# Bucketed attention, a routed expert layer and a dense layer: the third tile pair of each attention group split over two groups

## The chip, the cores and the metric

One core of a Trainium2 chip runs the whole program in one launch. The metric is the device time of that launch in microseconds (us). The kernel before took 792.55 us in the median of three runs (791.42 to 792.79).

## The reference

Three layers follow each other.

```python
# attention: 2 x 8 heads, 768 tokens, 64 wide
q_bucket = sum(((q @ proj) > 0) * 2**arange(6))      # the same for k
scores = where(q_bucket == k_bucket, q @ k.T / 8, -1e9)
attn = exp(scores - max(scores)); attn /= sum(attn) + 1e-9
x = attn @ v                                          # 1536 tokens x 512
# expert layer: 8 experts, the best one of each token, 512 -> 1024 -> 512
# dense layer: 512 -> 2048, ELU, -> 512
```

The change touches the attention alone.

## The kernel before

The work is written out by hand for each engine, with semaphores between the engines. `GROUPS` = 54 groups `n` are run; `g = n // 3` is the head that is being prepared and `part = n % 3` the third of it. Below, "head group g" means the three parts of one g. In its three parts TensorE prepares head g, takes the scores of head g-1 and applies the weights of an older head to v. The steady head groups are g = 2 to 15; g = 16 and the two parts that follow (n = 51, 52) only finish what is under way, and the document calls them the drain.

A head has six query tiles of 128 rows, numbered through all heads as `m`. In part p of head group g the tiles `m_s` and `m_s + 1` get their scores, with `m_s = 2 * (n - 3)`, and the tiles `m_e = m_s - 2` and `m_e + 1` have their exponentials transposed. The steps, with the line of the profile that shows each:

- `scores(m)` (L1274, TensorE): four matmuls into `pair_s` (m even) or `pair_t` (m odd). It waits until `exp_rows(m - 2)` has read that buffer, and for all masks of its head.
- `row_max(m)` (L900, VectorE, writes `nmax`), then `exp_rows(m)` (L699, ScalarE, writes `exps`, with a short instruction that reads the accumulator behind it).
- `turn_exps(m)` (L1285, TensorE): six transposes into the two halves of `pair_u`, three and three. `copy_t0(m)` (L708, ScalarE) takes the first half to `exps_t`, `copy_t1(m)` (L929, VectorE) the second. Each half of `turn_exps(m)` waits for the copy of that half of tile m - 1.
- `times_v(u, half)` (L1300, TensorE): 12 matmuls of `exps_t` with v into `bank_b`. `last(u)` (L1320) then multiplies with the closing weights into the same `bank_b`, and `copy_rows(u)` (L731, ScalarE) empties it. `times_v(u, 0)` waits for `copy_rows(u - 1)`.
- preparation of q (c = 0) and k (c = 1) of head g, all through `bank_a`: `turn_qk` (L1238, TensorE), `split_hi` (L670/672, ScalarE), `split_lo` (L892, VectorE, writes `x_lo`), `project` (L1252, TensorE), `keep_low` (L690, ScalarE, writes `low_sb`), `sign` (L912, VectorE, writes `bits`), `code` (L1260, TensorE), and two masks, `mask_even` (L921, VectorE) and `mask_odd` (L680/683, ScalarE). `turn_qk` of the next one waits for both masks, since they read the same bank.

Each engine runs its steps strictly in the order written. On TensorE that is, in parts 1 and 2:

```
part 1: scores, scores, turn_qk(g,1), turn_exps(m_e), times_v, project(g,1), turn_exps(m_e+1)
part 2: scores, scores, code(g,1), turn_exps(m_e), last, turn_qk(g+1,0), turn_exps(m_e+1)
```

On VectorE part 2 is `copy_t1(m_e-1)`, `row_max(m_s)`, `mask_even(g,1)`, `row_max(m_s+1)`, `copy_t1(m_e)`. On ScalarE it is `copy_t0(m_e-1)`, `mask_odd(g,1)`, `copy_t0(m_e)`, `exp_rows(m_s)`, `exp_rows(m_s+1)`, `split_hi(g+1,0)`.

Of the kernel before, what the change touches and what calls it, by code (L numbers as in the profile page):

```python
# [39 lines left out]
HEADS = B * H  # L40
SCALE = D ** -0.5
J = S // P
# [85 lines left out]
def program(nc, q, k, v, proj, w_gate, w_ogate, w1, w2, w_in, w_out, const, out):  # L128
    with ExitStack() as ctx:
# [247 lines left out]
        def chunk_of(w, n, part, c):  # L377
            return w[:, n % 2, part, c * CHUNK:(c + 1) * CHUNK]
# [284 lines left out]
        def _(act):  # L663
            def split_hi(g, c):
                u = 2 * g + c
                if g >= 2:
                    act.wait_ge(s_sc, J * (g - 1))
                act.wait_ge(s_tqk, u + 1)
                if c == 0:
                    act.activation(tiles(q_b, g, 0), turned(prep_bank(u)), ACT.Copy).then_inc(s_hi, 1)  # L670
                else:
                    act.activation(tiles(k_b, g, 1), turned(prep_bank(u)), ACT.Copy, scale=SCALE).then_inc(s_hi, 1)
# [13 lines left out]
            def keep_low(g, c):  # L686
                u = 2 * g + c
                act.wait_ge(s_sgn, u - 1)
                act.wait_ge(s_bits, u + 1)
                act.activation(low_sb[0:D, c, :], prep_bank(u)[D:P, 0:HALF], ACT.Copy).then_inc(s_low, 1)  # L690

            def exp_rows(m):
                (g, qt), u = place_of(m), unit_of(m)
                act.wait_ge(s_mx, m + 1)
                if u >= 4 and m % J == JH:
                    act.wait_ge(s_x, u - 3)
                if m >= 4:
                    act.wait_ge(s_pt, 2 * (m - 3))
                act.activation(exps[:, m % 4, :].rearrange("p (h n) -> p h n", h=2), score_pair[m % 2][:, :, 0:HALF],  # L699
                               ACT.Exp, bias=nmax[:, g % 2, qt:qt + 1],  # L700
                               accum_out=den[:, u % 4, qt:qt + 1]).then_inc(s_ex, 1)

            def copy_t0(m):
                hh = m // JH
                if hh >= 4:
                    act.wait_ge(s_av, (hh - 1) // 2)
                act.wait_ge(s_pt, 2 * m + 1)
                act.activation(turned_tile(m, slice(0, JH)),  # L708
                               exps_pair(m)[:, 0, 0:HALF].rearrange("p (j n) -> p j n", j=JH), ACT.Copy).then_inc(s_t0, 1)
# [75 lines left out]
            for n in range(6, GROUPS):  # L785
                g, part = n // 3, n % 3
                m_s, m_e = 2 * (n - GROUP_S), 2 * (n - GROUP_E)
                if 0 <= m_e - 1 < J * HEADS - 1:
                    copy_t0(m_e - 1)
                if part == 0 and 3 <= g < HEADS + 2:  # L790
                    copy_rows(g - 3)
                if g < HEADS and part == 1:
                    split_hi(g, 1)
                if g < HEADS and part == 2:
                    mask_odd(g, 1)
                if 0 <= m_e < J * HEADS:
                    copy_t0(m_e)
                if g < HEADS and part == 0:
                    keep_low(g, 0)
                if m_s < J * HEADS:  # L800
                    exp_rows(m_s)
                    exp_rows(m_s + 1)
                if n == 3 * HEADS + 3:
                    copy_t0(m_e + 1)
                if g >= 2 and part == 1:
                    copy_u(g - 2)
                if g < HEADS and part == 1:
                    keep_low(g, 1)
                if g < HEADS and part == 0:
                    mask_odd(g, 0)  # L810
                if g + 1 < HEADS and part == 2:
                    split_hi(g + 1, 0)
# [30 lines left out]
            for blk in range(BLOCKS):  # L843
# [6 lines left out]
                for f in range(FT + 1):  # L850
                    if f < FT:
                        n = blk * FT + f
# [15 lines left out]
        def _(dve):  # L868
# [46 lines left out]
            def mask_even(g, c):  # L915
                u = 2 * g + c
                if g >= 2:
                    dve.wait_ge(s_sc, J * (g - 1))
                dve.wait_ge(s_code, u + 1)
                to = tiles(k_a, g, 0)[D:P] if c else tiles(q_a, g, 0)[D:P]  # L920
                dve.tensor_scalar(to, turned(prep_bank(u))[0:D], popcount[0:D, :], BIG if c else -1.0,  # L921
                                  ALU.is_equal, ALU.mult if c else ALU.add).then_inc(s_mq, 1)

            def copy_t1(m):
                hh = m // JH
                if hh >= 4:
                    dve.wait_ge(s_av, (hh - 1) // 2)
                dve.wait_ge(s_pt, 2 * m + 2)
                dve.tensor_copy(turned_tile(m, slice(JH, J)),  # L929
                                exps_pair(m)[:, 1, 0:HALF].rearrange("p (j n) -> p j n", j=JH)).then_inc(s_t1, 1)  # L930
# [39 lines left out]
            for n in range(6, GROUPS):  # L970
                g, part = n // 3, n % 3
                m_s, m_e = 2 * (n - GROUP_S), 2 * (n - GROUP_E)
                if 0 <= m_e - 1 < J * HEADS:
                    copy_t1(m_e - 1)
                if g < HEADS and part == 0:
                    split_lo(g, 0)
                if m_s < J * HEADS:
                    row_max(m_s)
                if g < HEADS and part == 2:
                    mask_even(g, 1)  # L980
                if m_s < J * HEADS:
                    row_max(m_s + 1)
                if g < HEADS and part == 1:
                    split_lo(g, 1)
                if 0 <= m_e < J * HEADS:
                    copy_t1(m_e)
                if g < HEADS and part == 0:
                    sign(g, 0)
                if g < HEADS and part == 0:
                    mask_even(g, 0)  # L990
                if n == 9:
                    dve.wait_ge(s_cst, 16)
                    dve.tensor_copy(tri_bf[:, :], cc("tri"))
                    dve.tensor_copy(ones_bf[:, :], cc("ones"))
                    dve.tensor_copy(iota_bf[:, :], cc("iota"))
                if part == 1 and g >= 2:
                    inverse(g - 2)
                if part == 1 and 8 <= g < 8 + NCH:
                    dve.wait_ge(s_wld[g - 8], 16)
                    dve.tensor_copy(chunk_of(w_part, 0, 0, g - 8), w_raw[0][g - 8][:, :]).then_inc(s_whi, 1)  # L1000
                if g < HEADS and part == 1:
                    sign(g, 1)

# [223 lines left out]
        def _(pe):  # L1227
# [27 lines left out]
            def code(g, c):  # L1255
                u = 2 * g + c
                pe.wait_ge(s_sgn, u + 1)
                if u == 0:
                    pe.wait_ge(s_setup, 1)
                pe.matmul(prep_bank(u)[:, 0:HALF], pat_bf[:, :], bits[:, c, :], start=True, stop=True).then_inc(s_code, 1)  # L1260
# [110 lines left out]
            for n in range(6, GROUPS):  # L1371
                g, part = n // 3, n % 3
                m_s, m_e = 2 * (n - GROUP_S), 2 * (n - GROUP_E)
                if m_s < J * HEADS:
                    scores(m_s)
                    scores(m_s + 1)
                if g < HEADS and part == 1:
                    turn_qk(g, 1)
                if g < HEADS and part == 2:
                    code(g, 1)  # L1380
                if 0 <= m_e < J * HEADS:
                    turn_exps(m_e)
                if g < HEADS and part == 0:
                    project(g, 0)
                if n == 3 * HEADS + 3:
                    turn_exps(m_e + 1)
                if g == 2 and part == 0:
                    times_v_alone(0, 0, 0)
                if g >= 3 and part <= 1:
                    times_v(g - 2, part)  # L1390
                if n == 3 * HEADS + 4:
                    times_v_alone(HEADS, HEADS - 1, 2 * HEADS - 1)
                if g == 2 and part == 2:
                    last_alone(0)
                if g >= 3 and part == 2:
                    last(g - 2)
                if n == 3 * HEADS + 5:
                    last_alone(HEADS)
                if g < HEADS and part == 0:
                    code(g, 0)  # L1400
                if g < HEADS and part == 1:
                    project(g, 1)
                if g + 1 < HEADS and part == 2:
                    turn_qk(g + 1, 0)
                if 0 <= m_e < J * HEADS and n != 3 * HEADS + 3:
                    turn_exps(m_e + 1)


            def warm(stage):
# [188 lines left out]
```

## Time and profile before

| what | value |
|---|---|
| median of three runs | 792.55 us |
| the profiled execution | 792.53 us |
| its span, first to last instruction | 790.7 us |
| TensorE matmul busy | 770.2 us (97%) |
| VectorE busy | 453.1 us (57%) |
| ScalarE busy | 371.5 us (47%) |
| GpSimd busy | 341.4 us (43%) |
| mean granted TensorE clock | 0.999 of full speed |

The span is what the trace covers; the execution is 1.83 us longer than it. Busy shares are averages over the whole span, and the attention is its first third, up to about 264 us. A timeline row gives the start, the length, the engine, the line, the operation with output and inputs, and the count of merged instructions; in brackets stands the idle time of the engine before it and what ended that.

### The profile page before, as it was taken

What the parts mean: (1) busy time and instruction counts of PE and PEld (TensorE: products, weight loads), DVE (VectorE), ACT (ScalarE), POOL (GpSimd) and SP (SyncE); (2) the same over time, 40 slices, a digit from 0 to 9 for tenths busy, and PEclk for the clock granted to TensorE, in tenths of its full rate; (3) what the DMA queues carried; (4) which work ended last, traced back from release to release, by engine and by line L of the source; (5) the groups of instructions that cost most, each with busy time, mean ns of one, the idle gap of its engine ahead of it and who ended that gap; (6) DMA issues with size and microseconds to landing.
All of it is one profiled execution on the core that took longest, in us unless ns stands there. A gap on an engine that the chain in (4) does not pass through costs nothing.

```text
span 790.7 us, 12747 instructions
## 1 busy us (share of the span) xinstructions
PE 770.2 (97%) x4269; PEld 645.6 (82%) x4269; DVE 453.1 (57%) x805; ACT 371.5 (47%) x702; POOL 341.4 (43%) x340
## 2 busy tenths in 40 slices
PE   8899999999999999999999999999999999999997
PEld 5777777777777678888888888899899889989985
DVE  7777777788777664454444544669337316613720
ACT  6777777877786242134331340067227206503610
POOL 4344344655563289897777982134210010000000
PEclk9999999999999999999999999999999999999999
DMA  6022332231110187576465740430010020000000
GB/s 200 22 63 68 110 91 68 69 80 41 42 32 11 42 317 243 196 240 220 167 210 177 240 160 27 163 131 1 27 54 1 2 66 14 0 14 28 1 14 27
DMA packets 41805, 72.68 MB, mean 92 GB/s; under 512 B 18768, under 2 KB 25168, under 8 KB 41744
## 3 DMA queue, kind: packets, MB, share of 16 engines
q10 hardware_dynamic: 9456, 31.53, 12.0%
q1 hardware_dynamic: 28848, 29.06, 11.8%
q0 software_dynamic: 3440, 11.28, 4.4%
q8 instruction: 38, 0.62, 0.3%
q14 instruction: 23, 0.19, 0.1%
HBM read 60.57 MB, written 11.28 MB: 91 GB/s over the span
## 4 chain that ended last, share of the span: by engine, by line
PE 54%; issue 30%; DVE 9%; ACT 3%; POOL 2%; DMA 0%; POOLq 0%; ACTq 0%; DVEq 0%
PE pair_s L1470 13%; PE pair_t L1485 13%; PE bank_b L1300 8%; PE pair_u L1285 5%; DVE nmax L900 3%; PE pair_s L1274 3%; PE pair_t L1274 3%; PE pair_u L1449 2%; DVE exps_t L929 2%; PE bank_a L1252 2%; POOL out L642 1%; PE pair_s L1522 1%; DVE g_lo L1217 1%; ACT low_sb L690 1%; POOL y_raw L636 1%
## 5 line engine op out<-in xcount | busy, mean ns | idle before, releaser
L472 POOL TENSOR_TENSOR w_part<-w_raw,w_part 128x1024 fp32r<-128x1024 f32 x80 | 190.2, 2407 | 57.3 <-ACT w_part L750 56.6
L750 ACT ACTIVATE w_part<-w_raw 128x1024 fp32r<-128x1024 f32 x72 | 73.9, 1055 | 133.8 <-PE pair_t L1485 99.9
L1572 PE MATMUL pair_t<-w_part,g_hi 128*128 128x512 f32 x384 | 119.0, 391 | 0.3 <-POOL w_part L472 0.3
L1470 PE MATMUL pair_s<-w_part,xs_t 128*128 x456 | 108.7, 394 | 0.4 <-DVE xs_t L1095 0.4
L1485 PE MATMUL pair_t<-w_part,hid_t 128*128 x456 | 109.0, 394 | 0.0
L642 POOL DMA_INDIRECT out<-o_sb,token x12 | 11.8, 987 | 208.4 <-DVE o_sb L1187 208.4
L1470 PEld LDWEIGHTS pair_s<-w_part,xs_t 128*128 128x128 f32 x456 | 84.2, 188 | 17.7 <-issue 0.9
L1485 PEld LDWEIGHTS pair_t<-w_part,hid_t 128*128 128x128 f32 x456 | 84.4, 189 | 16.8
L854 ACT ACTIVATE elu<-elu 128x384 f32<-128x384 f32 x64 | 33.6, 525 | 123.2 <-DVE elu L1207 123.0
L1285 PE MATMUL pair_u<-first,exps 128*128 128x128 f32 x564 | 80.5, 274 | 6.0 <-DVE exps_t L929 5.7
L1572 PEld LDWEIGHTS pair_t<-w_part,g_hi 128*128 128x128 f32 x384 | 71.6, 188 | 15.1 <-issue 0.7
L1285 PEld LDWEIGHTS pair_u<-first,exps 128*128 128x128 f32 x564 | 65.9, 140 | 12.9 <-DVE exps_t L929 9.3
L1572 PE MATMUL pair_t<-w_part,g_lo 128*128 128x512 f32 x192 | 74.9, 390 | 0.0
L1522 PE MATMUL pair_u<-y_t,w_part 128*128 128x384 f32 x384 | 69.3, 334 | 0.3 <-DVE elu L1212 0.3
L1522 PE MATMUL pair_s<-y_t,w_part 128*128 128x384 f32 x384 | 69.3, 335 | 0.0
L1522 PEld LDWEIGHTS pair_u<-y_t,w_part 128*128 128x128 f32 x384 | 66.8, 188 | 0.7 <-DVE elu L1212 0.6
L1522 PEld LDWEIGHTS pair_s<-y_t,w_part 128*128 128x128 f32 x384 | 66.9, 188 | 0.2
L1113 DVE CAST hid_t<-pair_u 128x512 fp32r<-128x512 f32 x38 | 26.0, 685 | 67.2 <-PE pair_u L1449 67.2
L1300 PE MATMUL bank_b<-exps_t,v_nat 128*64 128x384 f32 x360 | 64.5, 494 | 0.1
L929 DVE COPY exps_t<-pair_u 128x384 f32<-128x384 f32 x94 | 51.6, 549 | 15.1 <-PE pair_u L1285 14.5
L708 ACT ACTIVATE exps_t<-pair_u 128x384 f32<-128x384 f32 x94 | 46.2, 491 | 15.5 <-PE pair_u L1285 14.4
L1104 DVE TENSOR_SCALAR hid<-pair_s 128x1024 f32<-128x1024 f32 x19 | 23.3, 1224 | 46.8 <-PE pair_s L1470 46.8
(233 smaller groups left out, 1231.4 us busy)
## 6 DMA issues: line engine op xcount, KB each, us to landing
w_raw<-in_moe_w ACTq DMA_DIRECT2D x48, 512.0 KB, 3.9
w_raw<-in_moe_w SPq DMA_DIRECT2D x16, 512.0 KB, 8.3
ys_sorted<-ys SPq DMA_DIRECT2D x19, 256.5 KB, 6.0
w_raw<-in_moe_w_in ACTq DMA_DIRECT2D x8, 512.0 KB, 4.1
raw<-in_q SPq DMA_DIRECT2D x16, 192.0 KB, 3.6
raw<-in_k SPq DMA_DIRECT2D x16, 192.0 KB, 3.5
v_nat<-in_v SPq DMA_DIRECT2D x16, 192.0 KB, 2.4
x_rows<-rows_sb SPq DMA_DIRECT2D x32, 96.0 KB, 2.4
```

Of the source, the lines that this page charges most:

```text
L472: pool.tensor_tensor(chunk_of(w_part, n, 1, c), w_raw[n % 2][c][:, :], chunk_of(w_part, n, 0, c).bitcast(F32), ALU.subtract).then_inc(s_wl ...
L708: act.activation(turned_tile(m, slice(0, JH)), exps_pair(m)[:, 0, 0:HALF].rearrange("p (j n) -> p j n", j=JH), ACT.Copy).then_inc(s_t0, 1)
L750: act.activation(chunk_of(w_part, n, 0, c), w_raw[n % 2][c][:, :], ACT.Copy).then_inc(s_whi, 1)
L854: act.activation(elu[:, n % 3, :], elu[:, n % 3, :], ACT.Exp).then_inc(s_em, 1)
L929: dve.tensor_copy(turned_tile(m, slice(JH, J)), exps_pair(m)[:, 1, 0:HALF].rearrange("p (j n) -> p j n", j=JH)).then_inc(s_t1, 1)
L1274: mm = pe.matmul(score_pair[m % 2][:, h, 0:HALF], a[:, g % 2, t], b[:, g % 2, h * HALF:(h + 1) * HALF], start=first, stop=not first)
L1285: mm = pe.transpose(exps_pair(m)[:, part, n * P:(n + 1) * P], exps[:, m % 4, kt * P:(kt + 1) * P], ident)
L1300: mm = pe.matmul(u_bank(u)[o * D:(o + 1) * D, 0:HALF], v_nat[:, (u - 1 + o) % 4, j, :], turned_half(2 * u - 1 + o)[:, j], start=j == 0, st ...
L1470: mm = pe.matmul(pair_s[:, h, :], xs_t[:, xp, c * P:(c + 1) * P], w_part[:, bass.ds(par, 1), wp, a:a + 512], start=c == 0 and xp == 0 and ...
L1485: mm = pe.matmul(pair_t[:, s % 2, :], hid_t[:, hp, c * P:(c + 1) * P], w_part[:, bass.ds(par, 1), wp, a:a + DM], start=c == 0 and n == 0, ...
L1522: mm = pe.matmul(hidden_bank[n % 4][:, 0:NB], w_in_p[:, wp, c, f * P:(f + 1) * P], y_t[:, yp, c, :], start=c == 0 and m == 0, stop=c == CD ...
L1572: mm = pe.matmul(pair_t[:, t % 2, :], gp[:, f, j * P:(j + 1) * P], w_out_p[:, wp, f, :], start=f == 0 and m == 0, stop=f == FT - 1 and m == 2)
```

## The change

TensorE's part 1 takes the first score tile of part 2 with it, behind `times_v`; VectorE takes that tile's maximum in part 1 too, ahead of `sign(g,1)`. In part 2 VectorE's `mask_even(g,1)` goes behind `copy_t1(m_e)`, ScalarE's `mask_odd(g,1)` goes behind `copy_t0(m_e)` and the first `exp_rows` ahead of it, and TensorE's `turn_qk(g+1,0)` goes behind `turn_exps(m_e+1)`. In the drain (n = 51) `times_v(15, 0)` goes ahead of the two last `turn_exps`. No instruction is added or taken away.

```diff
 # ScalarE
+                if m_s < J * HEADS and part == 2:
+                    exp_rows(m_s)
+                if 0 <= m_e < J * HEADS:
+                    copy_t0(m_e)
                 if g < HEADS and part == 2:
                     mask_odd(g, 1)
-                if 0 <= m_e < J * HEADS:
-                    copy_t0(m_e)
                 if g < HEADS and part == 0:
                     keep_low(g, 0)
+                if m_s < J * HEADS and part < 2:
+                    exp_rows(m_s)
                 if m_s < J * HEADS:
-                    exp_rows(m_s)
                     exp_rows(m_s + 1)
...
 # VectorE
-                if m_s < J * HEADS:
+                if m_s < J * HEADS and part < 2:
                     row_max(m_s)
-                if g < HEADS and part == 2:
-                    mask_even(g, 1)
                 if m_s < J * HEADS:
                     row_max(m_s + 1)
...
                     copy_t1(m_e)
+                if g < HEADS and part == 2:
+                    mask_even(g, 1)
...
+                if part == 1 and m_s + 2 < J * HEADS:
+                    row_max(m_s + 2)
                 if g < HEADS and part == 1:
                     sign(g, 1)
...
 # TensorE
+                if m_s < J * HEADS and part < 2:
+                    scores(m_s)
                 if m_s < J * HEADS:
-                    scores(m_s)
                     scores(m_s + 1)
...
+                if n == 3 * HEADS + 3:
+                    times_v(g - 2, 0)
                 if 0 <= m_e < J * HEADS:
                     turn_exps(m_e)
...
-                if g >= 3 and part <= 1:
+                if g >= 3 and part <= 1 and n != 3 * HEADS + 3:
                     times_v(g - 2, part)
+                if part == 1 and m_s + 2 < J * HEADS:
+                    scores(m_s + 2)
...
+                if 0 <= m_e < J * HEADS and n != 3 * HEADS + 3:
+                    turn_exps(m_e + 1)
                 if g + 1 < HEADS and part == 2:
                     turn_qk(g + 1, 0)
-                if 0 <= m_e < J * HEADS and n != 3 * HEADS + 3:
-                    turn_exps(m_e + 1)
```

## Rows read from the trace of the kernel before

**Rows 1.** Busy time by engine in one steady head group (g = 8).
```profile
115.46:131.16 15.70, 15.34 (x106) 11.76 (x104) 12.64 (x21) 12.23 (x27) 6.86 (x13) 1.00 0.33 100
```

**Rows 2.** TensorE's waits over the span: total us, times, longest us.
```profile
PE pair_u L1285 <- DVE exps_t L929: 5.7, 14, 0.6
```

**Rows 3.** Timeline of TensorE, from the end of times_v in part 1 to that head group's end.
```profile
125.52 0.44 PE L1252 MATMUL bank_a<-k_b,proj_w 128*128 128x384 f32 x1
125.80 0.34 PE L1252 MATMUL bank_a<-x_lo,proj_w 128*128 128x384 f32 x1
125.97 0.82 PE L1285 MATMUL pair_u<-first,exps 128*128 128x128 f32 x6
126.55 0.59 PE L1274 MATMUL pair_s<-k_a,q_a 128*128 128x384 f32 x2
126.98 0.51 PE L1274 MATMUL pair_s<-k_b,q_b 128*128 128x384 f32 x2
127.33 0.51 PE L1274 MATMUL pair_t<-k_a,q_a 128*128 128x384 f32 x2
...
128.03 0.34 PE L1260 MATMUL bank_a<-bits,pat_bf 128*128 128x384 bf16 x1
128.20 0.82 PE L1285 MATMUL pair_u<-first,exps 128*128 128x128 f32 x6
128.85 0.98 PE L1320 MATMUL bank_b<-last_w,u_sb 128*128 128x160 f32 x6
129.67 0.49 PE L1238 MATMUL bank_a<-first,raw 128*128 128x128 f32 x3
130.00 0.49 PE L1285 MATMUL pair_u<-first,exps 128*128 128x128 f32 x3
130.86 0.33 PE L1285 MATMUL pair_u<-first,exps 128*128 128x128 f32 x1 [0.36 <-DVE exps_t L929]
```

**Rows 4.** Timeline of VectorE, the same stretch.
```profile
126.83 0.55 DVE L912 SCALAR_TENSOR_TENSOR bits<-bank_a,low_sb 64x384 bf16<-64x384 f32 x1 [1.04 <-ACT low_sb L690]
127.30 0.54 DVE L929 COPY exps_t<-pair_u 128x384 f32<-128x384 f32 x1
127.76 0.94 DVE L900 TENSOR_REDUCE nmax<-pair_s 128x1 f32<-128x768 f32 x1
128.74 0.61 DVE L921 TENSOR_SCALAR k_a<-bank_a,first 64x384 fp32r<-64x384 f32 x1
129.38 0.96 DVE L900 TENSOR_REDUCE nmax<-pair_t 128x1 f32<-128x768 f32 x1
130.25 0.55 DVE L929 COPY exps_t<-pair_u 128x384 f32<-128x384 f32 x1
```

**Rows 5.** Timeline of ScalarE, keep_low in the same stretch.
```profile
126.23 0.49 ACT L690 ACTIVATE low_sb<-bank_a 64x384 f32<-64x384 f32 x1
```

**Rows 6.** Timeline of VectorE at the start: a copy and a mask behind it.
```profile
20.01 0.55 DVE L929 COPY exps_t<-pair_u 128x384 f32<-128x384 f32 x1
20.59 0.61 DVE L921 TENSOR_SCALAR k_a<-bank_b,first 64x384 fp32r<-64x384 f32 x1
```

**Rows 7.** Timeline of TensorE, head group 2, part 1: project(2,1).
```profile
30.03 0.44 PE L1252 MATMUL bank_a<-k_b,proj_w 128*128 128x384 f32 x1 [0.70 <-DVE x_lo L892]
```

**Rows 8.** Timeline of ScalarE in the drain: exp_rows(95), copy_t0(93), copy_rows(14).
```profile
254.26 0.91 ACT L699 ACTIVATE exps<-pair_t,nmax 128x768 f32<-128x768 f32 x1
...
255.13 0.49 ACT L708 ACTIVATE exps_t<-pair_u 128x384 f32<-128x384 f32 x1
255.50 0.59 ACT L731 ACTIVATE rows_sb<-bank_b 128x480 f32<-128x480 f32 x1
```

**Rows 9.** Timeline of TensorE in the drain: turn_exps(91), then times_v(15).
```profile
250.30 0.87 PE L1285 MATMUL pair_u<-first,exps 128*128 128x128 f32 x6
...
254.64 0.82 PE L1285 MATMUL pair_s<-first,exps 128*128 128x128 f32 x6
...
256.24 4.09 PE L1300 MATMUL bank_b<-exps_t,v_nat 128*64 128x384 f32 x24
```

## The prediction
> **What bounds the kernel now.** I read the busy time by stretch first. In a steady head group TensorE is busy 15.34 us of 15.70, VectorE 12.64 and ScalarE 12.23 [rows 1]. So TensorE sets the pace, with a hole in it. The list of its waits names the hole: 14 waits, 5.7 us in all, for VectorE's copy of the second half of `pair_u` [rows 2]; there are 14 steady head groups. The timeline shows where it lies: at the end of part 2 the second half of `turn_exps(m_e+1)` starts at 130.86, though the first half began at 130.00 [rows 3]. A whole `turn_exps` takes 0.58 (125.97 to 126.55), half of one 0.29, so the second half could have started at 130.29. The hole is worth 0.57 us of issue time a head group, more than the 0.36 shown in the bracket, because the ends of matmuls are modelled. The reader is to see in VectorE's rows why: `row_max`, `mask_even`, `row_max` and only then `copy_t1(m_e)`, 130.25 to 130.80, and TensorE 0.06 behind it [rows 4]. The two maxima can't be earlier, since their scores are only taken in part 2. All later work starts from the end of the attention, so a microsecond saved here is one saved at the end.
>
> **The change, part by part.** I rebuild the stretch of [rows 3] in the new order, keeping the start of project at 125.52 as the start of the moved scores.
>
> TensorE. One `scores` behind another kind takes 0.78 (126.55 to 127.33), a `project` behind a `times_v` 0.45 (125.52 to 125.97), of which 0.11 is the change of kind (0.28 between its two matmuls, against 0.17 elsewhere); behind scores I take 0.34 [rows 3]. The moved scores run 125.52 to 126.31, project to 126.65, `turn_exps(m_e+1)` to 127.23, the one score tile left to 128.01. Nothing is added: the kind changes as often as before. The moved scores need `exp_rows` of the same part, which was over by then: no row of [rows 3] shows a wait for it.
>
> VectorE, the new long chain. The moved `row_max` starts when its scores end, 0.43 + 0.51 + 0.05 = 0.99 behind their start [rows 3], at 126.51, and leaves VectorE at 127.38 (0.87 from one start to the next, 129.38 to 130.25 [rows 4]). But now `sign(g,1)` stands behind it, and behind the later project: second matmul at 126.48, `keep_low` 0.43 later (125.80 to 126.23 [rows 3, 5]), `sign` 0.60 behind that (to 126.83 [rows 4, 5]), so `sign` starts at 127.51. Then, with the spacings of [rows 4]: `copy_t1(m_e-1)` +0.47 = 127.98, `row_max` +0.46 = 128.44, `copy_t1(m_e)` +0.87 = 129.31, and `mask_even` +0.58 (a copy and a mask behind it, 20.01 to 20.59 [rows 6]) = 129.89, over at 130.50.
>
> Back on TensorE. `code(g,1)` needs `sign`: 127.51 + 0.55 + 0.06 = 128.12, a new wait of 0.11. `turn_exps(m_e)` 128.29 (its second half at 128.58 needs `copy_t1(m_e-1)`, over at 128.53, plus 0.06: just met), `last` 128.94 (0.65 later, as 128.20 to 128.85), `turn_exps(m_e+1)` 0.82 later at 129.76. Its second half at 130.05 needs `copy_t1(m_e)`, over at 129.86: the hole is closed. It is done at 130.34. Late next is `turn_qk(g+1,0)`: it needs the mask, over at 130.50, so 130.58 with 0.08 for the signal, and 0.33 later (129.67 to 130.00 [rows 3]) the next head group starts: 130.91 against 131.16 before (130.86 plus 0.30). The gain is 0.25 us a head group. TensorE alone would have been ready at 130.56, which bounds the gain at 0.60. The other end: if every start on VectorE in the new chain waits for the end of the instruction before it, the chain grows by 4 x 0.03 plus the four overlaps (0.08, 0.08, 0.09, 0.08), near 0.4 with rounding, and the head group gets 0.1 to 0.2 us longer than before. I take 0.25, since these very spacings are in [rows 4].
>
> ScalarE. The first `exp_rows` of part 2 now comes ahead of `copy_t0(m_e)`. That copy is wanted at 129.76; its input is there at 128.88 (0.59 behind 128.29), so 0.3 us is in hand. If exp came later than that, the hole would come back in the first half. `mask_odd`, behind it, ends near 130.0, ahead of VectorE's mask. The copy of turned q, `split_hi`, now starts 0.26 behind the new group's first scores, as late as before within 0.1, since `turn_qk` has moved with the rest; the preparation that follows has its old distance to TensorE. GpSimd's placing of k waits for `project` and is some 0.8 us later, and is needed over 3 us later still. No DMA is in the moved steps, and SP's loads wait for an older `turn_qk` that doesn't move.
>
> Three head groups differ. In g = 2 there is no `times_v` in part 1, and TensorE stood 0.70 for `x_lo` ahead of project [rows 7]; the moved scores fill that, so I take 0.70 there (bounds 0.25 and 1.1). In g = 15 there is no `turn_qk` behind, the next scores need the mask alone: 130.50 + 0.06, a gain of 0.60. The 12 between give 12 x 0.25 = 3.0. Together 4.3 us.
>
> The drain costs some of it. `times_v(15, 0)` writes the bank that `last(14)` filled, so it waits for `copy_rows(14)`, which on ScalarE stands behind `exp_rows(95)` and `copy_t0(93)` [rows 8]. Before, the last two `turn_exps` (254.64 on [rows 9]) filled TensorE's time until then, and it began at 256.24, 0.74 behind `copy_rows`. After, on the same clock: the moved scores of tile 94 start when `times_v` ends, 250.30; `turn_exps(91)` 251.09; scores of 95 at 251.67; its maximum 0.99 later and 0.96 long, exp near 253.78 (254.26 before), `copy_rows` near 255.02, `times_v` at 255.76. That is 0.48 earlier. But the two `turn_exps` (2 x 0.58) now come behind it, with 0.18 for going back to `times_v`: 0.48 - 1.34, a loss of 0.86, and 0.14 for the tail of a `times_v` that no longer runs straight into the next. TensorE stands over 1 us for `copy_rows`. I take a loss of 1.0 (bounds 0 and 1.4).
>
> The sum: 0.7 + 3.0 + 0.6 - 1.0 = 3.3 us less than the profiled execution's 792.53 (span 790.7 and 1.83 around it), which is the median of the runs within 0.02: **789.2 us**.
>
> A rule bears on the spacing. In [rows 4] `copy_t1` starts 0.87 behind a maximum that lasts 0.96, but `mask_even` 0.98 behind one of 0.94. The Trainium skill, "VectorE: DVE Perf Modes", section "Two Vector instructions with no wait between them", says that an instruction whose output begins in another quadrant of partitions than the last output is held until all earlier ones are over; the masks write the upper 64 partitions, and the trace agrees. The same page's "The DRAIN you can't avoid" says that after every operation "the next op does not start until the 8-stage pipe empties". By that one alone the four spacings above would be full lengths and the gain would be gone; the trace disagrees for the copies.
>
> **The rivals.**
>
> A. As above: the hole closes, VectorE's chain sets a smaller one at `turn_qk`, the drain loses 1.0. Own range 788.0 to 790.5 (the head group's gain 0.15 to 0.35, the drain by 0.4).
>
> B. TensorE becomes the bound. The chain on VectorE is quicker than I lay it, and the hole goes whole: 12 x 0.60 + 1.1 + 0.6 - 1.0 = 7.9, near 784.7. For it: only 0.35 us of slack is missing. Against it: every spacing has a row.
>
> C. The wait is handed on: the chain through the late `project`, `keep_low`, `sign` ends no earlier than it did, and `turn_qk` takes the hole over. With the head group's gain between 0 and 0.1: 0.7 + 0.6 + 0.6 - 1.0 = 0.9 at the middle, 791.6; same. For it: 0.25 is small beside a chain of eight steps. It covers too that the change doesn't do what it says, the copy of the second half still being late.
>
> D. Slower. One mechanism: VectorE's chain from the moved maximum to the mask loses its overlaps, because each of its instructions now comes to a wait that is only just met (`sign` and `copy_t1` above). From 0.25 us of growth a head group on, the steady part gains nothing; at the 0.4 of the bound above it is 12 x -0.15 + 0.3 + 0.2 - 1.0 = -2.3, or 794.8. For it: `copy_t1(m_e-1)` and `turn_exps` meet within 0.05. Against it: behind the waiting `sign` at 126.83 the next copy still came 0.47 later, with its overlap.
>
> **How the numbers follow.** A 0.62, B 0.09, C 0.15, D 0.14. A measurement of this kernel can tell 0.2%, 1.6 us, from no change: faster means under 791.0, slower over 794.1. A and B are faster, and 0.04 of C: 0.75. The other 0.11 of C and 0.06 of D, where the chain grows by less, are within: 0.17. Slower keeps 0.08. The range takes in A whole, C and the quicker side of D, and half of what lies toward B: 786.0 to 792.8.
>
> **What would show it.** In the changed trace: no wait of `turn_exps` for `exps_t`; in its place about 0.2 us ahead of `turn_qk`, ended by VectorE's `k_a`, and 0.1 ahead of `code`; a steady head group of 15.45 us; `times_v(15)` behind an idle TensorE of a microsecond, released by `copy_rows`. The prediction is wrong if the head group is under 15.25 or over 15.6, if ScalarE's `copy_t0` ends the waits in place of VectorE, or if the drain is no longer than before.

## The result and the profile after

The changed kernel took 789.22 us in the median of five runs (787.79 to 789.62), the kernel before 792.00 beside it (791.42 to 792.79). The ratio is 0.9958, 95% interval 0.9944 to 0.9973: 0.42% faster, clear of no change. The forecast was 789.2 of 792.53. That the two figures for the changed kernel agree within 0.02 us is luck: its five executions lie 1.8 us apart, the medians differ by 2.8 us (3.3 by the ratio) where 3.3 was forecast, and in the next table one row is off by 0.6 us and another by 0.2 the other way. The profiled executions have spans of 787.8 and 790.7 us (the changed kernel's is the slowest of its five), at a granted clock of 0.999 in both.

Cut by the starts of TensorE's work, the two traces hardly differ behind the attention:

| stretch | before | after | difference | forecast |
|---|---|---|---|---|
| start to head group 2 | 21.25 | 21.88 | +0.63 | 0 |
| head group 2 | 15.62 | 14.89 | -0.73 | -0.7 |
| head groups 3 to 14 | 188.45 | 185.22 | -3.23 | -3.0 |
| head group 15 | 15.70 | 15.11 | -0.59 | -0.6 |
| drain, to the start of `last(15)` | 21.17 | 22.25 | +1.08 | +1.0 |
| all the rest | 528.49 | 528.42 | -0.07 | 0 |

The first line is taken as not the change's: the instructions of that stretch are written out ahead of the loop and are the same in both kernels, and 0.46 of the 0.63 is there when the very first `scores` starts (9.71 before, 10.17 after). Without it the traces differ by 3.5 us. One thing speaks against: over all twelve traces the stretch took 21.15 to 21.29 us in the four kernels without the moved scores and 21.30 to 21.91 in the eight with them. Why is open, so part of the 0.63 may belong to the change after all.

VectorE in the same stretch of the same head group as [rows 4], in the kernel after:

```profile
125.03 0.96 DVE L903 TENSOR_REDUCE nmax<-pair_s 128x1 f32<-128x768 f32 x1 [0.75 <-PE pair_s L1279]
126.03 0.55 DVE L915 SCALAR_TENSOR_TENSOR bits<-bank_a,low_sb 64x384 bf16<-64x384 f32 x1
126.50 0.54 DVE L932 COPY exps_t<-pair_u 128x384 f32<-128x384 f32 x1
126.97 0.94 DVE L903 TENSOR_REDUCE nmax<-pair_t 128x1 f32<-128x768 f32 x1
127.83 0.54 DVE L932 COPY exps_t<-pair_u 128x384 f32<-128x384 f32 x1
128.40 0.61 DVE L924 TENSOR_SCALAR k_a<-bank_a,first 64x384 fp32r<-64x384 f32 x1
```

And TensorE, as [rows 3]:

```profile
124.03 0.62 PE L1279 MATMUL pair_s<-k_a,q_a 128*128 128x384 f32 x2
124.48 0.51 PE L1279 MATMUL pair_s<-k_b,q_b 128*128 128x384 f32 x2
124.83 0.34 PE L1257 MATMUL bank_a<-k_b,proj_w 128*128 128x384 f32 x1
...
125.75 0.59 PE L1279 MATMUL pair_t<-k_a,q_a 128*128 128x384 f32 x2
...
126.64 0.34 PE L1265 MATMUL bank_a<-bits,pat_bf 128*128 128x384 bf16 x1
126.81 0.83 PE L1290 MATMUL pair_u<-first,exps 128*128 128x128 f32 x6
127.48 0.98 PE L1325 MATMUL bank_b<-last_w,u_sb 128*128 128x160 f32 x6
128.30 0.82 PE L1290 MATMUL pair_u<-first,exps 128*128 128x128 f32 x6
129.12 0.52 PE L1243 MATMUL bank_a<-first,raw 128*128 128x128 f32 x3
129.39 0.59 PE L1279 MATMUL pair_s<-k_a,q_a 128*128 128x384 f32 x2
```

The reader is to see two things. The last `turn_exps` (128.30) is one merged row of six: its second half no longer waits, where it was two rows 0.86 apart on [rows 3]. And `turn_qk` starts at 129.12, 0.82 behind it, where 0.65 is the pace, and 0.11 behind the end of the mask at 129.01: that is the new wait, some 0.16 us, though no bracket shows it, since the modelled ends of matmuls cover gaps of that size. Counted from the start of the moved scores, the steps stand so:

| step | forecast | measured |
|---|---|---|
| moved `row_max` | 0.99 | 1.00 |
| `sign` | 1.99 | 2.00 |
| `copy_t1(m_e-1)` | 2.46 | 2.47 |
| `row_max` | 2.92 | 2.94 |
| `copy_t1(m_e)` | 3.79 | 3.80 |
| `mask_even` | 4.37 | 4.37 |
| `turn_qk` | 5.06 | 5.09 |
| next head group | 5.39 | 5.36 |

A steady head group is 15.435 us (185.22 / 12), against 15.704. The list of TensorE's waits from 17 to 264 us lost the line of [rows 2] and shows two new ones:

```profile
PE pair_s L1279 <- ACT exps L699: 1.5, 1, 1.5
PE bank_b L1305 <- ACT rows_sb L731: 0.9, 1, 0.9
```

The first is head group 2, where no `times_v` covers the time until `exp_rows(8)` frees the buffer; it took the place of the 0.70 of [rows 7] and of the hole, and the group still gained. The second is the drain:

```profile
250.10 0.82 PE L1290 MATMUL pair_u<-first,exps 128*128 128x128 f32 x6
251.78 2.16 PE L1305 MATMUL bank_b<-exps_t,v_nat 128*64 128x384 f32 x12 [0.87 <-ACT rows_sb L731]
253.87 0.87 PE L1290 MATMUL pair_s<-first,exps 128*128 128x128 f32 x6
254.58 0.82 PE L1290 MATMUL pair_t<-first,exps 128*128 128x128 f32 x6
255.33 2.16 PE L1305 MATMUL bank_b<-exps_t,v_nat 128*64 128x384 f32 x12
```

`turn_exps(93)` is issued by 250.68, `times_v(15, 0)` starts at 251.78, and the two `turn_exps` that stood ahead of it on [rows 9] come only then. `copy_rows(14)` starts 0.71 ahead of `times_v`, as on [rows 8, 9] (0.74). Counted from the start of head group 16, `times_v(15, 0)` starts 0.54 earlier than before (14.68 against 15.22), where 0.48 was forecast:

```profile
249.76 0.90 ACT L699 ACTIVATE exps<-pair_t,nmax 128x768 f32<-128x768 f32 x1
...
250.69 0.49 ACT L708 ACTIVATE exps_t<-pair_u 128x384 f32<-128x384 f32 x1
251.07 0.56 ACT L731 ACTIVATE rows_sb<-bank_b 128x480 f32<-128x480 f32 x1
```

### The profile page after: what moved, and what is told of

The parts are those of the page before. It is cut to its first block, busy times and chain, and to the rows that moved or that the text cites. A ratio compares the mean times of both kernels' runs of the same rounds, so it can differ in the third digit from the quotient of the medians.

```text
span 787.8 us, 12747 instructions
## 1 busy us (share of the span) xinstructions
PE 772.6 (98%) x4269; PEld 646.3 (82%) x4269; DVE 453.6 (58%) x805; ACT 372.9 (47%) x702; POOL 340.7 (43%) x340
## 4 chain that ended last, share of the span: by engine, by line
PE 63%; issue 28%; DVE 4%; POOL 2%; ACT 2%; DMA 0%; POOLq 0%; DVEq 0%; ACTq 0%
PE pair_s L1480 13%; PE pair_t L1495 13%; PE bank_b L1305 8%; PE pair_u L1290 7%; PE pair_s L1279 5%; PE pair_t L1279 4%; PE pair_u L1459 2%; PE bank_a L1243 2%; PE bank_b L1325 1%; PE bank_a L1257 1%; POOL out L642 1%; PE pair_s L1532 1%; DVE g_lo L1222 1%; PE bank_a L1265 1%; POOL y_raw L636 1%
## 5 line engine op out<-in xcount | busy, mean ns | idle before, releaser
L1290 PE MATMUL pair_u<-first,exps 128*128 128x128 f32 x564 | 77.5, 273 | 0.3 <-ACT exps_t L708 0.2
L903 DVE TENSOR_REDUCE nmax<-pair_s 128x1 f32<-128x768 f32 x48 | 45.8, 954 | 18.0 <-PE pair_s L1279 17.0
```

Source lines behind the costliest of these rows:

```text
L903: dve.tensor_reduce(nmax[:, g % 2, qt:qt + 1], score_pair[m % 2][:, :, 0:HALF], AX.XY, ALU.max, negate=True).then_inc(s_mx, 1)
L1290: mm = pe.transpose(exps_pair(m)[:, part, n * P:(n + 1) * P], exps[:, m % 4, kt * P:(kt + 1) * P], ident)
```

## The experiments

The theory: the moved scores close the hole, VectorE's chain from the moved `row_max` to `mask_even` sets the steady head group, and the new drain order costs a microsecond. The rivals: the order of the masks does it; TensorE's own work sets the pace; the drain order is neutral. "Drain" in the table is the stretch of the table above, from head group 16 to the start of `last(15)`. All ratios are to the kernel before on the same chip; a "group" is the mean of head groups 3 to 14.

| kernel | ratio (95%) | group, us | drain, us |
|---|---|---|---|
| before | 1 | 15.70 | 21.2 |
| the change | 0.9958 (0.9944 to 0.9973) | 15.43 | 22.2 |
| e1 old drain order | 0.9940 (0.9926 to 0.9953) | 15.43 | 21.0 |
| e2 scores only | 0.9977 (0.9968 to 0.9986) | 15.58 | 21.2 |
| e3 order only | 1.0010 (1.0000 to 1.0019) | 15.74 | 21.8 |
| e4 drain order only | 1.0020 (1.0010 to 1.0029) | 15.70 | 22.8 |
| e5 one more copy in the chain | 1.0034 (1.0021 to 1.0048) | 15.90 | 22.2 |
| e6 the same copy in idle time | 0.9961 (0.9948 to 0.9974) | 15.47 | 22.2 |
| e7 one step of `last` twice | 0.9971 (0.9961 to 0.9981) | 15.52 | 22.2 |
| e8 a copy on ScalarE, old drain | 0.9936 (0.9922 to 0.9949) | 15.36 | 21.1 |
| e9 order only, ScalarE's old | 0.9984 (0.9974 to 0.9993) | 15.60 | 21.4 |
| e10 ScalarE's old order, old drain | 0.9967 (0.9954 to 0.9979) | 15.55 | 21.4 |

**e1: the old drain order.**

```diff
-                if n == 3 * HEADS + 3:
-                    times_v(g - 2, 0)
-                if g >= 3 and part <= 1 and n != 3 * HEADS + 3:
+                if g >= 3 and part <= 1:
                     times_v(g - 2, part)
```

> The changed kernel with the drain in its old order: times_v(15, 0) behind the two last turn_exps. Theory (the new drain order costs about 1 us, since times_v(15, 0) stands for copy_rows(14) while the two turn_exps that could fill the time come behind it): from the start of head group 16 to the end of the last times_v 20.8 us, against 22.2 in the changed kernel and 21.2 before, no wait of times_v for copy_rows over 0.2 us; the whole 1.4 us under the changed kernel, near 787.8. Rival (the new order is neutral or helps): the drain stays within 0.3 of the changed kernel's, or grows. The steady head group stays 15.43.

787.48 us, ratio 0.9940. The drain is 21.0 us, 1.25 less than in the change; the whole is 1.7 us less by the medians and 1.4 by the ratios, where 1.4 was expected. `copy_rows` stands where it did, but TensorE now has its two `turn_exps` to do meanwhile, and `times_v` follows at 252.15 without a wait:

```profile
250.09 0.82 PE L1290 MATMUL pair_u<-first,exps 128*128 128x128 f32 x6
250.75 0.82 PE L1290 MATMUL pair_s<-first,exps 128*128 128x128 f32 x6
251.40 0.82 PE L1290 MATMUL pair_t<-first,exps 128*128 128x128 f32 x6
252.15 4.09 PE L1305 MATMUL bank_b<-exps_t,v_nat 128*64 128x384 f32 x24
```

**e4: the drain order alone,** on the kernel before (the inverse of e1's edit).

> The kernel before with the new drain order alone. Theory: times_v(15, 0) still starts about 0.74 behind copy_rows(14), at the same distance from the start of head group 16 (15.2), and the two turn_exps come behind it: the stretch from the start of group 16 to the end of the last times_v grows from 21.2 to 22.6 us, the whole by 1.4, near 793.4, with TensorE idle for 1.3 us ahead of times_v. Rival (neutral): within 0.3.

794.07 us, ratio 1.0020: slower. The drain is 22.8 us, 1.6 more than before, with this wait of TensorE:

```profile
256.24 2.16 PE L1300 MATMUL bank_b<-exps_t,v_nat 128*64 128x384 f32 x12 [1.43 <-ACT rows_sb L731]
```

It starts at the very time of [rows 9]: the time is set by `copy_rows`, not by what TensorE did before. Both together settle the drain.

**e2: scores and their maximum only.** On e1's kernel:

```diff
 # ScalarE, VectorE: masks, copies and exp in the order before the change
 # TensorE
+                if g + 1 < HEADS and part == 2:
+                    turn_qk(g + 1, 0)
                 if 0 <= m_e < J * HEADS and n != 3 * HEADS + 3:
                     turn_exps(m_e + 1)
-                if g + 1 < HEADS and part == 2:
-                    turn_qk(g + 1, 0)
```

> Only the moved scores and their row_max; masks, turn_qk and the drain as before the change. Theory (VectorE's chain ends the head group): mask_even at 128.56 and row_max behind it on the clock of the forecast, copy_t1(m_e) at 130.07, turn_exps done at 130.98, so a steady head group of 15.51 (before 15.70, changed 15.43); the wait of turn_exps for exps_t is back, about 0.3 issue us each. In all 2.2 + 0.6 in group 2 + 0.2 in group 15 + 0.4 in the drain = 3.4 under the kernel before, near 788.7. Rival (the masks' order is what closes the hole): 15.70 a head group, only 0.5 to 1 us under the kernel before.

790.53 us, ratio 0.9977. A group takes 15.58 as a mean; eleven of the twelve take 15.55, one 15.92 (below). The wait of `turn_exps` is back: its two halves start at 129.40 and 129.97, 0.57 apart where 0.33 is the pace, and with the slower start of the second half some 0.3 a group is lost. The single group is within 0.04 of the expectation (15.51); the whole, 1.8 us, is little over half of the 3.4 expected. The drain gained nothing (21.23 us, before 21.17), the one slow group cost 0.37, and the stretch ahead of head group 2 was 0.35 longer. The moved scores alone give 0.12 a group as a mean, 0.15 without the slow one, of the 0.27 of the change.

**e3: the order only,** on the kernel before.

```diff
 # ScalarE: exp_rows(m_s), copy_t0(m_e), mask_odd, exp_rows(m_s + 1)
 # VectorE: row_max, row_max, copy_t1(m_e), mask_even
 # TensorE: turn_exps(m_e + 1), turn_qk(g + 1, 0)
```

> Only the order of masks, exp and turn_qk in part 2; scores, row_max and the drain as before the change. Theory: both maxima still come in part 2, copy_t1(m_e) at 129.50, the mask from 130.08 to 130.69, turn_qk at 130.77 and the next head group at 131.10: 15.64 a steady head group (before 15.70), a gain of 0.7 + 0.4 in group 15, some 1.2 us in all, near 790.8; the wait has gone from turn_exps to turn_qk. Rival (the masks' order is what closes the hole): 15.45 or less.

793.03 us, ratio 1.0010, and 15.74 a group: longer than before, where both guesses said shorter. The expectation reckoned VectorE's chain right (the mask starts at 130.09, expected at 130.08) and forgot ScalarE:

```profile
128.76 0.90 ACT L699 ACTIVATE exps<-pair_s,nmax 128x768 f32<-128x768 f32 x1 [1.50 <-DVE nmax L903]
129.56 0.19 ACT L699 ACTIVATION_READ_ACCUMULATOR exps<-pair_s,nmax 128x1 f32 x1
129.65 0.48 ACT L708 ACTIVATE exps_t<-pair_u 128x384 f32<-128x384 f32 x1
```

With the scores still in part 2, the maximum is late, ScalarE stands 1.50 us for it, and `copy_t0(m_e)`, queued behind, keeps TensorE waiting:

```profile
130.27 0.85 PE L1288 MATMUL pair_u<-first,exps 128*128 128x128 f32 x6 [0.42 <-ACT exps_t L708]
```

**e9: the same without ScalarE's part.**

```diff
 # ScalarE of e3 back to: mask_odd, copy_t0(m_e), exp_rows(m_s), exp_rows(m_s + 1)
```

> The kernel with only the order of part 2 changed, but ScalarE left in its old order (mask_odd, copy_t0(m_e), then both exp_rows). Theory (with both maxima in part 2, ScalarE's first exp_rows can't start before 128.7 and copy_t0(m_e) behind it ends near 130.1, 0.5 late for turn_exps; that made the order alone 15.74 a head group): without it VectorE's chain sets the group, mask_even over at 130.69, turn_qk 0.11 behind, the next group 0.27 later: 15.60 to 15.64, 12 x 0.1 + 0.4 in group 15, 1.3 to 1.6 us under the kernel before; no wait of turn_exps for ScalarE. Rival (ScalarE's order is not the cause): 15.74 again and no gain.

791.37 us, ratio 0.9984, 15.60 a group, and no wait for ScalarE in the steady groups. That confirms the cause of e3's miss. VectorE and TensorE at the end of the same head group:

```profile
128.83 0.54 DVE L929 COPY exps_t<-pair_u 128x384 f32<-128x384 f32 x1
129.40 0.61 DVE L921 TENSOR_SCALAR k_a<-bank_a,first 64x384 fp32r<-64x384 f32 x1
129.04 0.94 PE L1285 MATMUL pair_u<-first,exps 128*128 128x128 f32 x6
130.12 0.52 PE L1238 MATMUL bank_a<-first,raw 128*128 128x128 f32 x3
```

The wait of `turn_exps` is gone without the moved scores too: the masks' new order alone clears it and hands it to `turn_qk`, which follows the end of the mask (130.01) by 0.11. So the rival is right in part: this order alone gives 0.10 a group, the moved scores alone 0.12.

**e10: all of the change but ScalarE's order,** with the old drain.

```diff
 # ScalarE of the change back to: mask_odd, copy_t0(m_e), exp_rows(m_s), exp_rows(m_s + 1)
 # TensorE: the drain as in e1
```

> The changed kernel with the old drain order and ScalarE's old order in part 2. Theory (with the scores moved, VectorE's chain sets the group, and ScalarE has room either way: mask_odd behind code from 128.6 to 129.2, copy_t0(m_e) to 129.65, wanted at 129.76): 15.43 to 15.47 a head group, within 0.5 us of the same kernel with the new ScalarE order. Rival (the exp ahead of the copy is part of the gain): 15.55 or more, 1.5 us and over.

789.93 us, ratio 0.9967, 15.55 a group: the rival's number. VectorE's chain is untouched, and `turn_qk` follows the mask as before (129.20); but the two exps of part 2 start at 128.27 and 129.16 in place of 126.34 and 128.51 in the change (whose same steps come 0.08 earlier in the trace), `split_hi` is behind them, and the second score tile of the next group waits a moment for its buffer:

```profile
129.91 0.51 PE L1276 MATMUL pair_s<-k_b,q_b 128*128 128x384 f32 x2
130.29 0.59 PE L1276 MATMUL pair_t<-k_a,q_a 128*128 128x384 f32 x2
```

0.38 from one to the next, and 0.43 to the row after that (130.72), where 0.35 and 0.35 is the pace: 0.11 lost with hardly any idle time on record, which is nearly all of the 0.12 a group. The exp that reads this buffer, with its read of the accumulator, ends at 130.14, 0.15 ahead of the 130.29. So the edits of the steady part lean on each other: the moved scores give ScalarE an exp it can do early, and doing it early frees the buffer in time.

**e5 and e6: one more copy on VectorE,** to a spare buffer.

```diff
+                if again:
+                    dve.wait_ge(s_spare, spared[0])
+                    dve.tensor_copy(spare[:, :], exps_pair(m)[:, 1, 0:HALF]).then_inc(s_spare, 1)
+                    spared[0] += 1
...
-                    copy_t1(m_e - 1)
+                    copy_t1(m_e - 1, again=part == 2 and 3 <= g < HEADS)     # e5
-                    copy_t1(m_e)
+                    copy_t1(m_e, again=part == 1 and 3 <= g < HEADS)         # e6
```

> The changed kernel with one more VectorE copy of the same 128x384 tile, to a spare buffer that nothing reads, ahead of copy_t1(m_e-1) in part 2 of head groups 3 to 15: inside the chain from the moved row_max to mask_even. Theory (that chain sets the steady head group): each grows by the copy's full 0.46, 15.89 in place of 15.43, 5.5 to 6 us in all, near 795. Rival (TensorE's own work sets it): at most 0.1 each, 1 us in all.

> The changed kernel with the same additional copy, ahead of copy_t1(m_e) in part 1 of head groups 3 to 15, where VectorE stands idle for 0.75 us and more ahead of the moved row_max. Theory: nothing, 15.43 a head group and the whole within 0.5 us of the changed kernel. Rival (VectorE's total work counts): 15.89 as with the copy in the chain.

In the chain the copy costs its full 0.47 a group and 6.0 us in all (795.30, ratio 1.0034 against 0.9958); in the idle time nothing (789.45, ratio 0.9961). In e6's trace eleven groups take 15.43 to 15.46 and one, g = 6, takes 15.79; in e2 the same group is 0.37 longer than the others and in the kernel before 0.11. Each time one instruction of VectorE starts late in it (`sign` in e6 at 95.05, `mask_even` in e2 at 96.75 and before at 97.36); why stays open. Same engine, same instruction: what counts is the place. This is the plainest evidence that VectorE's chain sets the group. In e5:

```profile
128.26 0.55 DVE L917 SCALAR_TENSOR_TENSOR bits<-bank_a,low_sb 64x384 bf16<-64x384 f32 x1
128.74 0.54 DVE L938 COPY spare<-pair_u 128x384 f32<-128x384 f32 x1
129.20 0.54 DVE L940 COPY exps_t<-pair_u 128x384 f32<-128x384 f32 x1
```

TensorE meets the later copy at two places. The second half of `turn_exps(m_e)` now waits for it:

```profile
PE pair_u L1298 <- DVE exps_t L940: 3.5, 13, 0.3
131.00 0.82 PE L1298 MATMUL pair_u<-first,exps 128*128 128x128 f32 x6
131.81 0.52 PE L1251 MATMUL bank_a<-first,raw 128*128 128x128 f32 x3
```

But the group still ends with the mask: it is over at 131.71, and `turn_qk` starts at 131.81, 0.81 behind the last `turn_exps` as in the change, where its own pace would have let it start at 131.66.

**e7: one of the three steps of `last` twice** (two matmuls on record, 0.14 us each).

```diff
-                for i in range(JH):
+                for i in (0, 0, 1, 2) if u < HEADS - 2 else range(JH):
```

> The changed kernel with one of the three matmuls of last run twice in head groups 3 to 15 (it writes the same values again), 0.27 us more TensorE work each, 3.5 us in all. Theory (TensorE stands 0.24 ahead of turn_qk for VectorE's mask): nearly all of it is hidden, 15.43 to 15.47 a head group, under 0.6 us in all. Rival (TensorE's work sets the pace): 15.70, 3.5 us in all, near 792.7.

790.42 us, ratio 0.9971, 15.52 a group: 0.09 of the 0.27 shows, 0.18 is hidden. Neither guess is met: at most 15.47 was expected, and the rival (TensorE's work sets the pace) would have shown all of it. The room is 0.18, not 0.24; `turn_qk` follows without a wait, 0.66 behind the start of `turn_exps`, and TensorE is now the bound. The two are that close.

```profile
128.97 0.82 PE L1290 MATMUL pair_u<-first,exps 128*128 128x128 f32 x6
129.63 0.49 PE L1243 MATMUL bank_a<-first,raw 128*128 128x128 f32 x3
```

**e8: one of the chain's copies on ScalarE,** with the old drain order.

```diff
 # ScalarE, part 2 of head groups 2 to 15, behind copy_t0(m_e - 1)
+                if part == 2 and g < HEADS:
+                    copy_t1_act(m_e - 1)
 # VectorE
-                if 0 <= m_e - 1 < J * HEADS:
+                if 0 <= m_e - 1 < J * HEADS and not (part == 2 and g < HEADS):
                     copy_t1(m_e - 1)
```

> The changed kernel with the old drain order, and copy_t1(m_e-1) of part 2 of head groups 2 to 15 done by ScalarE behind its copy_t0(m_e-1) in place of VectorE: the chain on VectorE is one copy, 0.46, shorter. Theory: mask_even ends 0.46 sooner, TensorE's own work then sets the head group, 15.15 to 15.25, some 2.5 to 3.5 us under the changed kernel with the old drain alone, near 785. Rival (ScalarE takes the hole over, since exp and copy_t0(m_e) behind it come 0.4 to 0.8 later and copy_t0(m_e) had 0.3 us in hand): 15.4 or more, with waits of turn_exps for ScalarE's exps_t.

787.08 us, ratio 0.9936, the fastest, but within the error of e1. The group is 15.36, 0.08 less than e1's, where 0.2 or more was expected; neither guess is met. VectorE:

```profile
125.11 0.55 DVE L925 SCALAR_TENSOR_TENSOR bits<-bank_a,low_sb 64x384 bf16<-64x384 f32 x1
125.81 0.96 DVE L913 TENSOR_REDUCE nmax<-pair_t 128x1 f32<-128x768 f32 x1 [0.15 <-PE pair_t L1289]
126.81 0.56 DVE L942 COPY exps_t<-pair_u 128x384 f32<-128x384 f32 x1
127.41 0.61 DVE L934 TENSOR_SCALAR k_a<-bank_a,first 64x384 fp32r<-64x384 f32 x1
```

The copy that is gone left VectorE too early twice: `row_max` now waits for its scores (0.15), and `copy_t1(m_e)` comes 1.00 behind it, not 0.87, as its input leaves TensorE only then (`turn_exps(m_e)` starts at 125.89, held back by `code` behind `sign`, and the copy comes 0.92 behind it, as the next copy does behind its `turn_exps`: 127.36 to 128.29). The mask still ends last (128.02, `turn_qk` at 128.12): a shorter chain ran into the two that feed it.

## Why the prediction was right

**The hole and who closes it.** Right that it closes: the wait of [rows 2] is gone. No single edit does it all. The moved scores alone gain 0.12 a group and leave part of the wait (e2), the masks' order alone gains 0.10 and hands the wait to `turn_qk` (e9), the two together gain 0.15 (e10), and with ScalarE's order it is 0.27.

**VectorE's chain as the new bound.** Right to 0.03 us at every step, and by cause: e5 and e6. The overlaps taken from [rows 4] held, so rival D (overlaps lost) is out: `copy_t1` again starts 0.86 behind a `row_max` of 0.94, and the mask 0.57 behind a copy of 0.54. The Trainium skill's rule of held instructions ("VectorE: DVE Perf Modes", section "Two Vector instructions with no wait between them") agrees with both. The same page's sentence on the drain (section "The DRAIN you can't avoid"), which the prediction took by itself, would have made the chain 0.3 us longer, and the trace is against it for the copies; that section goes on to say that an instruction that is not held starts earlier, which the prediction left out. `sign` starts 0.59 behind `keep_low` (125.44 to 126.03), as the sum has it, but also 0.04 behind the end of `row_max` (125.99): the two paths meet there within 0.1 us, so this step bears out either. `turn_qk` came 0.03 later than laid out, and from there to the next scores it took 0.27 and not 0.33; together that is the 0.02 to 0.03 a group that the sum was short (0.2 us over 12 groups). The rival of the quick chain (B) is given near 784.7 in the prediction; its own terms give 792.53 - 7.9 = 784.6.

**The bound of TensorE's own work.** Of the right kind, too generous: 0.60 a group was given as the most that could be gained. Measured, the change took 0.27, e7 leaves 0.18 of room at `turn_qk`, and the wait for `sign` ahead of `code` is 0.1, so near 0.55 by this sum. No kernel here came to it: the shortest group is e8's, 0.35 under the kernel before.

**ScalarE.** The prediction said that it only had to be in time for `copy_t0(m_e)` and priced its edit at nothing. The sum was right, the view too narrow: e10 shows that its new order is worth 0.12 us a group, through the buffer that `exp_rows` frees, and e3 that the same order costs 0.14 a group (15.74 against 15.60) without the moved scores. The prediction took the whole change together, so neither showed in its number.

**Head groups 2 and 15.** 0.73 and 0.59 for 0.7 and 0.6. The reason given for group 2 was loose: the scores don't fill the time there, they wait 1.48 us for `exp_rows(8)`, and the gain comes from what no longer waits behind.

**The drain.** A loss of 1.08 for 1.0, by the mechanism named: e1 and e4.

What stays open: the profiled execution of e1 is 2.4 us shorter than that of the change, of which the drain explains 1.25. The remaining 1.1 lies in the dense layer, where the traces of e1 and e10 lack two short waits of TensorE (0.27 us for VectorE's `elu` and 0.34 for the weights' low part) that all the others have, e8 with the same drain as e1 among them. No run settles whether that goes with the kernel or with the execution. Open too are the longer stretch ahead of head group 2 and the slow group g = 6.

## What to carry to other kernels

When the engine that sets the pace waits for a copy, read what is queued ahead of that copy on its engine, and move the earliest thing that feeds the queue, here one tile of scores. Then lay out the whole chain from rows, with the start-to-start spacings and not the durations; it says where the next wait will be, and to a few hundredths of a microsecond. And look at every edit alone: one of the four here (the drain) lost a quarter of what the others gained, and another (ScalarE's order) is a loss or a gain by what the rest does. The scores and the masks' order are each worth only 0.10 to 0.12 a group alone.

## What the runs showed of the hardware

A wait of TensorE need not stand in a bracket: `turn_qk` stood some 0.16 us in the steady head group shown for the change, and the list of waits from 17 to 264 us has no line for it; it is read from start-to-start times. A matmul that starts late can cost more than its wait: in e10 the first two matmuls of a delayed score tile took 0.43 from their start to the next in place of 0.35, as they do behind another kind of matmul (129.39 to 129.82 in the change).
